# Attention and two MLPs on one core: the first two heads' loads and copies, and the order of the calls at the front and at both changes

## The chip, the cores and the metric

The kernel runs on one core of a Trainium2 chip. The metric is the device time of one launch in microseconds (us), as a median over runs. The launch computes everything, from the inputs in HBM to the output in HBM. The engines are TensorE (PE), VectorE (DVE), ScalarE (ACT), GpSimd (POOL) and SyncE (SP). Each has its own instruction stream, and they meet only in semaphores. SP issues nearly all DMAs, ACT a few.

## The reference

```python
# attention: q, k, v (2, 8, 768, 64), 16 centroids for each of 8 heads
q_assign = argmax(q_n @ c_n)          # nearest centroid of each query, on normed vectors
k_assign = argmax(k_n @ c_n)
mask = q_assign[:, :, :, None] == k_assign[:, :, None, :]
scores = where(mask, scale * q @ k.T, -1e9)
attn = exp(scores - max) / (sum + 1e-9)
x = (attn @ v) as (1536, 512)
# first MLP: w_in (512, 2048), w_out (2048, 512)
h = x @ w_in
x = where(h >= 1, h, where(h <= -1, 0, (h + 1) ** 2 / 4)) @ w_out
# second MLP: w_gate, w_val (512, 1536), w_out (1536, 512)
xn = x / sqrt(mean(x * x) + 1e-6) * rms_g
out = (silu(xn @ w_gate) * (xn @ w_val)) @ w_out
```

All is float32. There are 16 heads in all (2 batches by 8).

## The kernel before

**Numbers.** Matmuls take float32r. A value is split into a high part (a copy rounded to that type) and a low part (the difference), and a product is made from the high and low parts. The splitting is why each PSUM result is read twice: by ACT for the high part, by DVE for the low part.

**Attention, per head of 768 rows in 6 tiles.** Queries and keys of a head lie side by side in `nat` (128 rows by 128 columns a tile). `transpose_qk` transposes the six tiles into PSUM; ACT's `qk_high` writes the high part to `atile`, DVE's `qk_low` the low part to `btile`. In each, rows 0 to 63 are the queries (scaled and negated) and rows 64 to 127 the keys. `assign` multiplies them with the centroids; DVE's `assigned`, `hits` and `masks` and POOL's `rank` turn this into a one-hot mask, which `mask_t` transposes. `assemble` (SP) brings the operands of the scores together: four transfers for the high part (`assemble(True)`), two for the low part (`assemble(False)`), and `send_masks` two for the masks, eight a head, counted in `qk_assembled`. For head 0 ACT issues the low-part transfers (`first_assemble`), and its masks are copied by ACT and DVE without a transfer. `scores` computes one tile of scores, DVE's `cut` takes its extreme values, ACT's `exp` the exponential. `probs_t` transposes the result (nine units a head), `high` (ACT) and `low` (DVE) split it, and `pv` multiplies it with the values.

**Order.** Every engine's order is written out call by call in three places: the front (blocks -3 to 1), the tail of attention with the first steps of the first MLP, and the steps around the change to the second MLP. Between them run loops (`blk`, and `step`). In block n, `probs_t` and `pv` belong to head n, `scores(at(n), t)` to tile t+1 of head n+1 and for t=5 to tile 0 of head n+2, `mask_t`, `assemble` and `send_masks` to head n+2, `transpose_qk` and `assign` to head n+3, and `next_qk` loads head n+4.

**The start.** SP loads head 0's queries, then (`head0.behind()`) the RMS gain, the four pieces of the first up weights and the first down weights, and only then head 1 (which also waits for head 0's loads to land). ACT loads head 0's keys and then the centroids. PE runs `warm(7)`, the transpose of the centroids, `warm(3)`, the transposes of head 0, `warm(4)`, and head 0's assignment; `warm` multiplies ones with ones and its results are not used.

**The MLPs.** The steps run over both MLPs; step s has one pair of column blocks of the up product and one chunk of 512 tokens. An up product is made from seven partial products (`up_part(s, j)`, j = 0 to 6). They are added by DVE's `first_sum`, `second_sum`, `inner_first`, `inner_second`, `second_half` and `first_half` (semaphore `combined`) and ACT's `snap` and `copy_corner`. `bend` and `maximum` (first MLP) or `scale_gate`, `silu` and `product` (second) make the hidden values, `hidden_hi` and `hidden_lo` split them, and `down` multiplies them. PE's order is up(s), down(s-1). The up product's inputs for chunk c are sums of pieces of x, made by POOL (`second_t_sum`, `t_sum`) and split by ACT (`second_t_hi`, `t_hi`) and DVE (`second_t_lo`, `t_lo`). Steps 0 and 1 use chunk 0, steps 2 and 3 chunk 1, whose last parts need the last pair of heads. `up_part(s, 2)` waits for `first_half(s-1)`; `up_part(2, 1)`, `(2, 3)`, `(2, 5)` and `(2, 6)` wait for `second_t_lo` number 7, 8, 9 and 10. Steps 24 on are the second MLP; `take_y` (ACT or DVE) takes a finished down product out of PSUM, and `down` of the next chunk waits for that, one m at a time.

## Time and profile before

| | us |
|---|---|
| median of 3 runs | 818.58 (816.81 to 820.59) |
| the profiled execution | 821.07 |
| its span, first to last instruction | 819.2 |
| PE busy | 801.0 (98%) |
| DVE busy | 639.1 (78%) |
| ACT busy | 490.4 (60%) |
| POOL busy | 402.5 (49%) |

Times of rows are us from the start of the span. Attention fills it to about 270 us, the first MLP from there to about 535, the second the rest. The profiled execution is 1.9 us longer than its span. A busy PE may still be slow: the column PEclk is the clock granted to it, as a share of the full one.

### The profile page before, as it was taken

Reading aid. Unit: us, or ns where it says so; the run is one execution under the profiler, and the core shown is the slowest. Engines: PE = TensorE matmul, PEld = TensorE weight load, DVE = VectorE, ACT = ScalarE, POOL = GpSimd, SP = SyncE. Lnnn points to the kernel's source line nnn. Section 1 sums busy time; section 2 is a strip of 40 time slices with the busy share of each in tenths; the row PEclk is TensorE's granted clock in tenths of the full one; section 3 lists DMA queues with packets and bytes.
Section 4 is the critical chain, followed back from the end, with each engine's and each line's share of the span. In section 5 each row is a group of like instructions: output and inputs, shape, how many; then the busy total and the mean of one; then the engine's idle time right before and its main releaser. Section 6 shows DMA issues by size and latency. Waiting matters only on the chain.

```text
span 819.2 us, 15394 instructions
## 1 busy us (share of the span) xinstructions
PE 801.0 (98%) x5369; PEld 736.0 (90%) x5369; DVE 639.1 (78%) x1221; ACT 490.4 (60%) x894; POOL 402.5 (49%) x356
## 2 busy tenths in 40 slices
PE   7899999999999999999999999999999999999998
PEld 6799999999988889999999899898899999999997
DVE  5799999999997776575665678997767787878666
ACT  2888888888988676655555569877332222222221
POOL 1135443246568853652462465975393673919000
PEclk9999999999999989999999999999999999999999
DMA  8844754755641100200200110200220101110102
GB/s 187 194 108 113 168 131 114 160 125 123 140 109 46 37 1 27 78 1 27 70 8 27 34 45 27 65 26 2 65 66 2 52 1 52 39 27 27 48 31 78
DMA packets 65443, 54.83 MB, mean 67 GB/s; under 512 B 30080, under 2 KB 52608, under 8 KB 65376
## 3 DMA queue, kind: packets, MB, share of 16 engines
q1 hardware_dynamic: 64288, 53.33, 25.5%
q8 instruction: 39, 0.64, 0.3%
q10 hardware_dynamic: 1088, 0.62, 0.3%
q14 instruction: 28, 0.23, 0.1%
HBM read 27.30 MB, written 3.15 MB: 37 GB/s over the span
## 4 chain that ended last, share of the span: by engine, by line
PE 88%; DVE 3%; ACT 3%; DMA 2%; issue 2%; POOL 1%; SPq 1%; ACTq 0%; DVEq 0%; POOLq 0%
PE ps L921 34%; PE ps L949 14%; PE ps L961 12%; PE ps L752 8%; PE ps L735 8%; PE ps L702 4%; PE ps L705 4%; PE ps L770 1%; PE ps L793 1%; PE ps L794 1%; DMA k<-stage 1%; PE ps L816 1%; SPq L536 1%; DVE gl L1930 0%; DMA cnat<-in_centroids 0%
## 5 line engine op out<-in xcount | busy, mean ns | idle before, releaser
L921 PE MATMUL ps<-th,wh 128*128 128x256 f32 x840 | 240.9, 287 | 3.5 <-DVE hid L1904 2.7
L921 PE MATMUL ps<-tl,wh 128*128 128x256 f32 x840 | 239.2, 285 | 0.0
L921 PE MATMUL ps<-th,wl 128*128 128x256 f32 x840 | 239.1, 285 | 0.0
L921 PEld LDWEIGHTS ps<-th,wh 128*128 128x128 f32 x840 | 162.3, 193 | 7.6 <-DVE tl L1732 3.2
L921 PEld LDWEIGHTS ps<-tl,wh 128*128 128x128 f32 x840 | 162.4, 193 | 2.0
L921 PEld LDWEIGHTS ps<-th,wl 128*128 128x128 f32 x840 | 162.3, 193 | 0.0
L2419 POOL TENSOR_TENSOR wl<-wraw,wh 128x448 fp32r<-128x448 f32 x80 | 104.9, 1339 | 1.3
L1745 DVE TENSOR_SCALAR_CACHE_REDUCE sf<-ps 128x768 f32<-128x768 f32 x96 | 91.6, 955 | 15.2 <-PE ps L705 11.8
L1754 DVE TENSOR_TENSOR ptl<-ps,pth 128x512 fp32r<-128x512 f32 x144 | 94.7, 683 | 5.1 <-ACT pth L1163 4.9
L1163 ACT ACTIVATE pth<-ps 128x512 fp32r<-128x512 f32 x144 | 82.8, 588 | 24.8 <-PE ps L752 16.0
L2400 POOL TENSOR_TENSOR wraw<-corner,wraw 128x256 f32<-128x256 f32 x20 | 17.4, 869 | 153.9 <-DMA wraw<-in_moe_w_val 86.0
L1930 DVE TENSOR_TENSOR gl<-hid,gh 128x512 fp32r<-128x512 f32 x84 | 76.0, 910 | 20.1 <-ACT gh L1324 18.6
L1173 ACT ACTIVATE pbuf<-sf,minn 128x768 f32<-128x768 f32 x96 | 89.0, 928 | 1.6 <-DVE sf L1745 0.2
L1300 ACT ACTIVATE hid<-ps 128x256 f32<-128x256 f32 x60 | 22.8, 379 | 106.8 <-PE ps L921 106.8
L735 PE MATMUL ps<-ident,pbuf 128*128 128x128 f32 x576 | 80.6, 274 | 0.5 <-ACT pbuf L1173 0.5
L1913 DVE TENSOR_TENSOR hid<-hid,curve 128x512 f32<-128x512 f32 x48 | 42.6, 888 | 49.0 <-ACT curve L1315 49.0
L949 PE MATMUL ps<-gh,o1h 128*128 128x512 f32 x192 | 75.2, 392 | 0.0
L949 PE MATMUL ps<-gl,o1h 128*128 128x512 f32 x192 | 75.0, 391 | 0.0
L949 PE MATMUL ps<-gh,o1l 128*128 128x512 f32 x192 | 74.8, 390 | 0.0
L735 PEld LDWEIGHTS ps<-ident,pbuf 128*128 128x128 f32 x576 | 68.5, 141 | 6.9 <-DVE ptl L1754 0.7
L1324 ACT ACTIVATE gh<-hid 128x512 fp32r<-128x512 f32 x84 | 52.6, 628 | 36.4 <-DVE hid L1925 27.1
L752 PE MATMUL ps<-pth,vs 128*128 128x512 f32 x192 | 61.9, 363 | 0.0
(149 smaller groups left out, 1778.5 us busy)
## 6 DMA issues: line engine op xcount, KB each, us to landing
q<-atile SPq DMA_DIRECT2D x32, 192.0 KB, 3.4
k<-atile SPq DMA_DIRECT2D x32, 192.0 KB, 3.3
o1raw<-in_moe_w_out SPq DMA_DIRECT2D x8, 512.0 KB, 3.8
nat<-in_q SPq DMA_DIRECT2D x16, 192.0 KB, 4.0
wraw<-in_moe_w_in SPq DMA_DIRECT2D x24, 128.0 KB, 2.6
vnat<-in_v SPq DMA_DIRECT2D x16, 192.0 KB, 3.3
moved<-osb SPq DMA_DIRECT2D x16, 192.0 KB, 4.2
wraw<-in_moe_w_val SPq DMA_DIRECT2D x24, 128.0 KB, 2.6
```

What stands on the lines that cost most here:

```text
L735: last = pe.transpose(w[:, col + t * P:col + (t + 1) * P], pbuf[:, u, first + t, kt * P:(kt + 1) * P], ident[:, :])
L752: last = pe.matmul(ps_o[:, t0 // 4, 0:count * P], vs[:, u, kt, :], part[:, j % 3, col:col + count * P], start=(kt == 0 and i == 0), stop=( ...
L921: last = pe.matmul(dst[:, 0:HC], a[w][:, j, kt, :], b[c][:, j, kt, :], start=(opened and kt == 0 and i == 0), stop=(kt == KH - 1 and i == ...
L949: last = pe.matmul(bank(Y[m]), w[q % 2][:, e, o:o + P], x[b][:, e, :], start=(opens(s) and h == 0 and i == 0), stop=(closes(s) and h == 1 ...
L961: last = pe.matmul(bank(Y[m]), x[b][:, 0, m * P:(m + 1) * P], w[f][:, :], start=(opens(s) and i == 0), stop=(closes(s) and i == 2))
L1163: act.activation(pth[:, j % 3], wbank(PT_AT[j]), ACT.Copy).then_inc(probs_high, 1)
L1173: act.activation(pbuf[:, s, ts, :], sf[:, ts % 2, :], ACT.Exp, bias=minn[:, s, ts:ts + 1], scale=-1.0, accum_out=den[:, s, ts:ts + 1]).the ...
L1324: act.activation(gh[s % 2][:, e, :], half_of(s, e), ACT.Copy).then_inc(hidden_high, 1)
L1745: dve.tensor_scalar(two(sf[:, ts % 2]), score_slot(fixed, t)[:, :, 0:HALF], MASKED, None, ALU.min, ALU.min, accum_out=minn[:, s, ts:ts + 1 ...
L1754: dve.tensor_tensor(ptl[:, j % 3], wbank(PT_AT[j]), pth[:, j % 3].bitcast(F32), ALU.subtract).then_inc(probs_low, 1)
L1930: dve.tensor_tensor(gl[s % 2][:, e, :], half_of(s, e), gh[s % 2][:, e, :].bitcast(F32), ALU.subtract).then_inc(hidden_low, 1)
L2419: pool.tensor_tensor(lo[:, o], raw[:, o], hi[:, o].bitcast(F32), ALU.subtract).then_inc(up_split, 1)
```

## The change

- **Loads.** Head 0's queries and keys are loaded in halves of three tiles: SP loads the first halves (new semaphore `first_half_loaded`), ACT the second halves, behind the centroids. PE's first three transposes wait for the first halves alone. Head 1's load stands next on SP's queue and waits for the second halves.
- **Copies.** For heads 0 and 1 three of the four high-part transfers, those that stay on their partitions, become POOL instructions (`copies`, semaphore `first_copies`); one transfer remains. The scores of heads 0 and 1 and `qk_high` of heads 2 and 3 wait for them, and POOL's first `rank` stands behind all six.
- **Weights.** `head0.behind()` moves from the head of SP's queue to behind head 0's `send_masks`.
- **Orders.** The calls of all engines are reordered in the front; those of ACT, DVE, POOL and SP also at the change from attention to the first MLP (steps 0 to 6) and at the change to the second MLP (steps 19 to 33). `warm` goes from 7, 3, 4, 8 to 6, 0, 5, 2, 8.

The first hunks are SP's and PE's, then ACT's (both changes), DVE's (the first change), and POOL's.

```diff
         def whole(head, parity):
-            return filled(head, parity, DMAS) - (0 if parity else 2 * 16)
+            return filled(head, parity, DMAS) - (3 if parity else 5) * 16
...
-            sp.dma_start(nat[:, 0, :, 0:D], q_v[0]).then_inc(qk_loaded[0], 16)
+            sp.dma_start(nat[:, 0, 0:NT // 2, 0:D], q_v[0][:, 0:NT // 2, :]).then_inc(first_half_loaded, 16)
+            sp.dma_start(nat[:, 0, 0:NT // 2, D:P], k_v[0][:, 0:NT // 2, :]).then_inc(first_half_loaded, 16)
...
                         moves = ((q1[0:D, s], atile[0:D, s]), (k1[0:D, s], atile[D:P, s]),
                                  (k1[D:P, s], atile[D:P, s]), (q2[0:D, s], atile[0:D, s]))
+                        if fixed is not None and fixed < 0:
+                            moves = moves[1:2]
...
-            head0.behind()
             pre3.next_qk()
             pre2.assemble(True)
             pre2.next_qk()
             pre1.assemble(True)
+            pre1.next_v()
+            pre1.assemble(False)
             pre1.next_qk()
             pre2.behind()
-            head0.next_qk()
-            pre1.assemble(False)
             pre1.send_masks()
             head0.assemble(True)
-            pre1.next_v()
+            head0.next_qk()
             head0.assemble(False)
             head0.next_v()
             head0.send_masks()
+            head0.behind()
+            head1.assemble(True)
+            head1.move_half()
+            head1.assemble(False)
+            head1.next_v()
             head1.next_qk()
-            head1.next_v()
-            head1.assemble(True)
-            head1.assemble(False)
-            head1.move_half()
             head1.send_masks()
...
-            warm(7)
+            warm(6)
...
-            warm(3)
...
+                if ts == 0 and number in (0, 1):
+                    pe.wait_ge(first_copies, 3 * (number + 1))
...
-                pe.wait_ge(qk_loaded[s], filled(n + 3, s, 2))
+                if fixed == -3:
+                    pe.wait_ge(first_half_loaded, 2 * 16)
+                else:
+                    pe.wait_ge(qk_loaded[s], filled(n + 3, s, 2))
...
+                    if fixed == -3 and t == NT // 2:
+                        pe.wait_ge(qk_loaded[s], 2 * 16)
...
             transpose_qk(at(-3))
-            warm(4)
+            warm(5)
             assign(at(-3), FIRST)
             assign(at(-3), SECOND)
+            warm(2)
             transpose_qk(at(-2))
...
-            act.dma_start(nat[:, 0, :, D:P], k_v[0]).then_inc(qk_loaded[0], 16)
             act.dma_start(cnat[:, :], cent.rearrange("h c d -> (h c) d")).then_inc(centroids_loaded, 16)
+            act.dma_start(nat[:, 0, NT // 2:NT, 0:D], q_v[0][:, NT // 2:NT, :]).then_inc(qk_loaded[0], 16)
+            act.dma_start(nat[:, 0, NT // 2:NT, D:P], k_v[0][:, NT // 2:NT, :]).then_inc(qk_loaded[0], 16)
...
+                    if fixed in (-1, 0):
+                        act.wait_ge(first_copies, 3 * (fixed + 2))
...
             bend(0, 0)
             snap(1)
-            head16.spread_out()
+            second_t_hi(5, 1)
+            second_t_hi(6, 1)
             hidden_hi(0, 0)
             bend(0, 1)
+            head16.spread_out()
+            hidden_hi(0, 1)
+            bend(1, 0)
+            t_hi(2, 0, 1)
+            t_hi(2, 1, 1)
             copy_corner(1)
-            hidden_hi(0, 1)
-            second_t_hi(5, 1)
-            second_t_hi(6, 1)
             second_t_hi(7, 1)
-            bend(1, 0)
             second_t_hi(8, 1)
...
+            take_y(29, 3)
+            copy_corner(31)
             take_y(29, 2)
-            take_y(29, 1)
-            hidden_hi(30, 0)
-            snap(31)
-            copy_corner(31)
             silu(31)
-            take_y(29, 3)
...
             inner_second(1)
+            second_half(1)
             hidden_lo(0, 1)
             second_t_lo(4, 1)
-            second_half(1)
+            first_half(1)
             second_t_lo(5, 1)
             second_t_lo(6, 1)
             second_t_lo(7, 1)
+            maximum(1, 0)
             second_t_lo(8, 1)
-            maximum(1, 0)
+            first_sum(2)
             second_t_lo(9, 1)
-            first_half(1)
             second_t_lo(10, 1)
-            first_sum(2)
+            second_sum(2)
             hidden_lo(1, 0)
-            second_sum(2)
+            maximum(1, 1)
             inner_first(2)
             inner_second(2)
-            maximum(1, 1)
+            t_lo(2, 0, 1)
+            second_half(2)
             hidden_lo(1, 1)
-            second_half(2)
...
+                def copies():
+                    h, s = n + 2, u
+                    pool.wait_ge(qk_high_done, h + 1)
+                    if fixed == -2:
+                        pool.wait_ge(first_masks_cleared, 1)
+                    else:
+                        pool.wait_ge(first_copies, 3)
+                    for i, (dst, own) in enumerate(((q1, slice(0, D)), (k1, slice(D, P)), (q2, slice(0, D)))):
+                        if i:
+                            pool.wait_ge(first_copies, 3 * h + i)
+                        pool.tensor_scalar(dst[own, s], atile[own, s].bitcast(F32), 1.0, 0.0, ALU.mult, ALU.add)\
+                            .then_inc(first_copies, 1)
...
+                        if fixed == -2:
+                            pool.wait_ge(first_copies, 6)
...
+            pre2.copies()
+            pre1.copies()
             pre2.rank()
```

## Rows read from the trace of the kernel before

**Rows 1.** The page, part 1: busy us (share of the span) xinstructions.
```profile
PE 801.0 (98%) x5369; PEld 736.0 (90%) x5369; DVE 639.1 (78%) x1221; ACT 490.4 (60%) x894; POOL 402.5 (49%) x356
```
**Rows 2.** Windows: us, busy PE, PEld, DVE, ACT, POOL, PEclk, DMA share, GB/s.
```profile
20.00:30.00 10.00, 7.95 (x54) 6.87 (x54) 7.93 (x20) 8.29 (x14) 2.10 (x3) 1.00 1.00 200
30.00:40.00 10.00, 9.09 (x56) 8.64 (x57) 7.56 (x18) 7.20 (x13) 0.00 (x0) 0.83 0.83 207
...
100.00:200.00 100.00, 99.87 (x720) 93.06 (x719) 92.88 (x196) 84.57 (x159) 40.12 (x41) 1.00 0.54 125
...
500.00:550.00 50.00, 49.80 (x329) 45.57 (x328) 46.96 (x76) 39.05 (x71) 38.93 (x29) 1.00 0.17 49
550.00:600.00 50.00, 48.40 (x337) 44.53 (x335) 37.04 (x68) 26.74 (x51) 26.28 (x23) 1.00 0.10 28
```
**Rows 3.** Waits of PE: total us, times, longest us.
```profile
PE ps L921 <- DVE hid L1904: 2.7, 1, 2.7
...
PE ps L702 <- DMA k<-stage: 1.7, 1, 1.7
...
PE ps L961 <- ACT xr L1388: 1.0, 1, 1.0
```
**Rows 4.** The chain of waits over the first 60 us: start, us, what.
```profile
1.49 4.06 DMA cnat<-in_centroids
...
15.95 3.92 DMA nat<-in_k
...
25.50 5.38 DMA k<-stage
```
**Rows 5.** Timeline of the front: start, us, engine, line, output<-input, [idle before <-releaser].
```profile
9.79 1.59 PE L670 MATMUL ps<-ones 128*128 128x512 f32 x4
11.22 0.19 PE L793 MATMUL ps<-cb,atile 128*128 128x64 f32 x1
...
15.17 1.01 DVE L1788 SCALAR_TENSOR_TENSOR btile<-ps,fold,atile 128x768 fp32r<-128x768 f32 x1
...
18.23 0.62 PE L702 MATMUL ps<-k,q 128*128 128x384 f32 x2 [0.42 <-DMA q<-atile]
...
23.42 0.74 SPq L536 DMA_DIRECT2D q<-btile  x1
...
28.81 0.96 DVE L1745 TENSOR_SCALAR_CACHE_REDUCE sf<-ps 128x768 f32<-128x768 f32 x1 [0.41 <-ACT pbuf L1173]
...
30.91 0.82 PE L702 MATMUL ps<-k,q 128*128 128x384 f32 x2 [1.70 <-DMA k<-stage]
...
37.16 0.95 DVE L1745 TENSOR_SCALAR_CACHE_REDUCE sf<-ps 128x768 f32<-128x768 f32 x1
```
**Rows 6.** The source views of L2528 and L2549: duration ns min/median/max.
```profile
L2528 POOL TENSOR_SCALAR vs<-vnat x16: 505/512/523, 25.9 to 247.5; 128x384 fp32r<-128x384 f32 x16
...
L2549 POOL TENSOR_TENSOR tpair<-osb,moved x16: 1828/1847/2192, 55.0 to 276.5; 64x768 f32<-64x768 f32 x16
```
**Rows 7.** Timelines of DVE and ACT at the change to the first MLP.
```profile
282.06 2.39 DVE L1732 TENSOR_TENSOR tl<-traw,th 128x256 fp32r<-128x256 f32 x3
...
287.67 0.41 DVE L1904 TENSOR_TENSOR hid<-ps,snap 128x256 f32<-128x256 f32 x1
...
282.44 0.42 ACT L1152 ACTIVATE th<-traw 128x256 fp32r<-128x256 f32 x1 [1.93 <-POOL traw L2483]
```
**Rows 8.** Windows: the stretch behind the wait of 2.7 us.
```profile
290.00:295.00 5.00, 5.00 (x27) 4.91 (x26) 3.44 (x6) 2.10 (x4) 5.00 (x4) 0.60 0.01 2
```
**Rows 9.** The chain of waits at the change to the first MLP.
```profile
288.23 6.36 PE ps L921 x30
...
300.08 5.03 PE ps L921 x42
```
**Rows 10.** The source view of L1919, and the timeline of POOL.
```profile
L1919 DVE TENSOR_TENSOR hid<-hid,z x36: 683/693/1925, 531.7 to 809.4; 128x512 f32<-128x512 f32 x36
...
589.11 1.70 POOL L2410 TENSOR_SCALAR wh<-wraw 128x1792 fp32r<-128x1792 f32 x1
```

More of the change, by code:

```diff
@@ L623, in _ @@
             load_up(3)
+            load_up(4)
             load_out1(2)
-            load_up(4)
             load_out1(3)
@@ L1517, in _ @@
             t_hi(2, 3, 1)
+            hidden_hi(2, 0)
+            take_y(1, 2)
+            snap(3)
+            take_y(1, 3)
             t_hi(2, 4, 1)
-            take_y(1, 2)
-            hidden_hi(2, 0)
-            snap(3)
             bend(2, 1)
-            take_y(1, 3)
+            copy_corner(3)
+            t_hi(2, 5, 1)
             hidden_hi(2, 1)
-            t_hi(2, 5, 1)
+            bend(3, 0)
             t_hi(2, 6, 1)
-            copy_corner(3)
-            bend(3, 0)
             snap(4)
@@ L1553, in _ @@
             hidden_hi(6, 1)
+            take_y(5, 2)
             for s in range(7, 19):
@@ L1580, in _ @@
             t_hi(3, 1, 1)
-            t_hi(3, 2, 1)
             bend(21, 1)
@@ L1685, in _ @@
             silu(32)
+            hidden_hi(32, 0)
             snap(33)
-            hidden_hi(32, 0)
             copy_corner(33)
+            take_y(32, 0)
+            silu(33)
             take_y(32, 1)
-            silu(33)
             take_y(32, 2)
-            take_y(32, 0)
+            take_y(32, 3)
             hidden_hi(33, 0)
-            take_y(32, 3)
             for s in range(34, NS):
@@ L2041, in _ @@
             head0.low(6)
+            head0.cut(4)
             head0.low(7)
-            head0.cut(4)
-            head1.masks()
             head0.low(8)
             head0.cut(5)
+            head1.masks()
             head1.low(0)
@@ L2171, in _ @@
             maximum(5, 0)
+            maximum(5, 1)
             first_sum(6)
@@ L2174, in _ @@
             second_sum(6)
-            maximum(5, 1)
             inner_first(6)
@@ L2178, in _ @@
             second_half(6)
+            first_half(6)
             hidden_lo(5, 1)
-            first_half(6)
             take_y(5, 0)
+            maximum(6, 0)
             take_y(5, 1)
-            maximum(6, 0)
             maximum(6, 1)
@@ L2221, in _ @@
             take_y(19, 1)
+            take_y(19, 2)
             maximum(20, 1)
-            take_y(19, 2)
+            take_y(19, 3)
             add_squares(0, 0)
-            take_y(19, 3)
             first_sum(21)
             second_sum(21)
+            hidden_lo(20, 0)
             inner_first(21)
-            hidden_lo(20, 0)
+            inner_second(21)
             hidden_lo(20, 1)
-            inner_second(21)
             add_squares(0, 1)
@@ L2235, in _ @@
             first_half(21)
+            add_squares(0, 2)
+            t_lo(3, 1, 1)
             maximum(21, 0)
-            add_squares(0, 2)
-            maximum(21, 1)
             first_sum(22)
             second_sum(22)
+            maximum(21, 1)
+            hidden_lo(21, 0)
             inner_first(22)
-            t_lo(3, 1, 1)
-            hidden_lo(21, 0)
             inner_second(22)
+            hidden_lo(21, 1)
             second_half(22)
-            sums_lo(0)
-            hidden_lo(21, 1)
             t_lo(3, 2, 1)
-            first_half(22)
             t_lo(3, 3, 1)
             t_lo(3, 4, 1)
+            first_half(22)
+            t_lo(3, 5, 1)
+            sums_lo(0)
             maximum(22, 0)
-            t_lo(3, 5, 1)
+            take_y(21, 0)
+            take_y(21, 2)
+            take_y(21, 3)
+            take_y(21, 1)
             maximum(22, 1)
-            hidden_lo(22, 0)
-            take_y(21, 1)
             first_sum(23)
-            take_y(21, 2)
-            take_y(21, 0)
             second_sum(23)
             inner_first(23)
-            take_y(21, 3)
+            hidden_lo(22, 0)
+            inner_second(23)
             hidden_lo(22, 1)
-            inner_second(23)
+            second_half(23)
             inverse(0)
-            second_half(23)
             add_squares(1, 0)
-            add_squares(1, 1)
             first_half(23)
@@ L2271, in _ @@
             maximum(23, 0)
-            add_squares(1, 2)
+            maximum(23, 1)
+            add_squares(1, 1)
             first_sum(24)
@@ L2275, in _ @@
             second_sum(24)
-            maximum(23, 1)
+            hidden_lo(23, 1)
             inner_first(24)
             inner_second(24)
-            hidden_lo(23, 1)
             second_half(24)
+            scale_gate(24)
             first_half(24)
+            add_squares(1, 2)
             sums_lo(1)
-            scale_gate(24)
             t_lo(4, 0, 1)
             take_y(23, 1)
+            take_y(23, 3)
             take_y(23, 0)
@@ L2289, in _ @@
             second_sum(25)
+            hidden_lo(24, 0)
             take_y(23, 2)
             inner_first(25)
-            hidden_lo(24, 0)
             inner_second(25)
             second_half(25)
+            first_half(25)
             scale_gate(25)
-            take_y(23, 3)
+            product(25)
             t_lo(4, 1, 1)
-            first_half(25)
-            product(25)
             first_sum(26)
@@ L2328, in _ @@
             first_sum(28)
-            hidden_lo(27, 0)
             second_sum(28)
             inner_first(28)
+            inverse(2)
+            hidden_lo(27, 0)
             inner_second(28)
             second_half(28)
+            first_half(28)
             scale_gate(28)
@@ L2371, in _ @@
             product(31)
-            hidden_lo(31, 0)
             first_sum(32)
@@ L2376, in _ @@
             inner_second(32)
+            hidden_lo(31, 0)
             second_half(32)
```

322 lines of the change are left out of this document (161 added, 161 removed).

## The prediction

> **What bounds the kernel now.** I read the page first: TensorE (PE) is busy for 801.0 of 819.2 us [rows 1]. Only 18.2 us are idle, so anything worth microseconds must remove idle time of PE or time at its low clock. The windows say where both lie [rows 2]. From 100 to 200 us PE is busy 99.87 of 100, so a gain made ahead of it is carried through undiminished. From 20 to 40 us it is idle 2.05 + 0.91 us, and the granted clock in 30 to 40 is 0.83, which takes another 1.7 us (the granted clock is 1.00 at 2.4 GHz and 0.50 at 1.2); the 0.60 of 290 to 295 us [rows 8] shows the same at the change from attention to the first MLP. Third, PE's waits [rows 3] name the long ones: 2.7 us for DVE's L1904, 1.7 us for the mask transfer k<-stage, 1.0 us for ScalarE's L1388. The chain of waits over the front [rows 4] shows 5.38 us of that mask transfer, and 4.06 us of the centroid load ahead of everything.
>
> **Front: the start.** The centroid load is issued first on ScalarE's queue, in the slot that the K load has now (0.76 us instead of 1.49): its landing comes 0.7 us earlier, at about 4.8 us by the same 4.06 us [rows 4]. Two half loads follow it there and the other two halves go by SP; a whole load is there before the centroids are ready for PE, so I cost the halves at nothing. If a half landed a microsecond late, the first transposes would wait that long. With three warm matmuls gone, the transposes follow the centroid transpose at once. But five warm matmuls then stand ahead of the first assignment, still at the slow pace of the start (four now take 1.59 us [rows 5], five 2.0 from 8.2 on), so it starts at about 10.15 us instead of 11.22 [rows 5]: 1.1 us. The warm(2) added later delays head 1's transposes, whose ScalarE copy is awaited only by the DVE instruction at 15.17 [rows 5], 0.9 us after it is there: nothing.
>
> **Front: copies by GpSimd.** Six transfers of 192 KB of the first two heads become six tensor_scalar on 64 partitions by 768. No such row exists. The nearest is L2528, 128x384 in 0.51 us [rows 6]; twice the elements a partition give 1.0 us each. The bounds are 0.5 us (as if partitions counted) and 1.85 us (L2549, 64x768 with two inputs [rows 6]), 1.5 to 5.5 us for three. I take 3 us. Head 0's high part is whole at 8.9 us (the transposes end at 8.2, two ScalarE copies behind), so its copies run to 12. Its first scores come at 16.7: now 18.23 [rows 5], less the 1.1, less 0.4 of a wait for one of the removed transfers. Head 1's run from 13.7 to 16.7, its scores come after 27. Both are hidden, head 0's with 4.7 us to spare. Behind them on GpSimd waits only head 1's ranking, ready at about 17.4. ScalarE's copies for heads 2 and 3 also wait on them, and come at 18.5 and 26.
>
> Against this speaks a row: L1919 of DVE, two SBUF inputs, takes 0.69 us and once 1.93, beside a GpSimd tensor_scalar of 1.70 us [rows 10]. DVE's mask chain has four instructions with two SBUF inputs a head, 0.26 to 0.36 us each. If each start falls on a copy, each waits up to a copy; head 1's copies meet perhaps one or two of head 0's. I count 0.3 us, bounds 0 and 3. The Trainium skill ("SBUF — State Buffer", Who interferes with whom) says the shared port is an exclusive lock between GpSimd and a DVE instruction with two SBUF inputs, held for the whole instruction. L1919 agrees; by that rule alone the term would be a copy for every overlap.
>
> **Front: the queue.** Now SP issues head 1's low-part moves at 23.42 us, though their data is ready at 16.18 (15.17 + 1.01) [rows 5], because loads of heads 2, 3, 4 and v stand ahead. After the change they leave at about 15, head 2's load at about 10 instead of 15.22, and head 4's load behind the masks. Fewer issues and 1 MB of weights less ahead of 30 us shorten every landing. Head 2's K load, landing at 19.87 (15.95 + 3.92 [rows 4]), no longer holds the transposes of 20.00: they start at 17.6, 2.4 us earlier. From there ScalarE's table load and five exponentials run in the old order with hardly a gap, so the last cut of head 0, 28.81 + 0.96 = 29.77 us [rows 5], comes at about 27.35. The masks of head 1 are then long landed (sent at 22.5, landing by 27 even with the old 3.9), so the first scores of head 1 go at 27.45 instead of 30.91 [rows 5]: 3.5 us. The clock drop that now follows the wait of 30 us should go too, 1.7 us. But DVE then sets the pace: by its order the cut of head 1's second tile ends at 34.4 instead of 38.1 (37.16 + 0.95 [rows 5]), 3.7 us. PE has by then done one half assignment more. I take 4.3 less the 0.3 for the port: **4.0 us**. Bounds: 1.1 (only the start) and 5.2 (3.5 + 1.7).
>
> **Weights later.** Six issues of about 0.6 us leave SP behind head 2's masks, at about 31 to 35 us, so they end long before head 1's next move has its data (when PE has ended head 1's scores, after 40). GpSimd sums the first weights only behind head 1's work. Nothing; if the cover were gone, head 3's assembly would be late by 3.5 us at most.
>
> **First change, attention to MLP.** PE's order is the same. Now its up(2) stops before j=2 from 285.5 to 288.23 [rows 3, 9] because j=2 waits for first_half(1), which DVE runs at 287.67, behind six second_t_lo and maximum(1, 0) [rows 7]; its products were done before down(0) began. Then PE runs 30 matmuls in 6.36 us, where 42 take 5.03 us later [rows 9], so 2.8 us go to the clock. In the new order first_half(1) stands behind second_t_lo(4), at about 282. What is late next is j=1: second_t_lo(7) needs the attention output, and ScalarE does bend(1, 0), two t_hi and a corner ahead of its part, so its copy at 282.44 [rows 7] comes at 283.7; j=1 starts at 284.95 instead of 284.5. j=3 waits for second_t_lo(8) behind maximum(1, 0), to 286.95; j=5 and j=6 for the next two, to 289.05. up(2) ends at 289.8 instead of 294.59. down(1) then loses about 1.1 us at its second half (hidden_lo(1, 1) at 293.6). Left: 4.8 - 1.1, **3.6 us** rounded down. It holds only if pieces of idle of 0.5 to 1.1 us do not lower the clock as 2.74 us did. Bounds: 0.8 (clock falls as before) and 5.5 (stall and clock all gone). The spreading of reciprocals is moved behind bend(0, 1), to 279.0; GpSimd's multiplication needs it at 278.88: 0.1 us, inside.
>
> **Second change, MLP to MLP.** PE is idle 0.2 us in 500 to 550 and 1.6 in 550 to 600 (49.80 of 50, 48.40 of 50 [rows 2]). The largest is the 1.0 us wait for ScalarE's L1388 [rows 3]: take_y(29, 3) stands behind silu(31), which waits for the stretched L1919. In the new order take_y(29, 2) and (29, 3) stand ahead of silu(31): 1.0 us off. The rest of the reordering I cannot price but by these rows: **1.0 us**, bounds 1.8 off and 1.5 more, since DVE is busy 46.96 of 50 us there [rows 2]. Attention's loop and the last stages are untouched.
>
> **Sum.** 4.0 + 3.6 + 1.0 = 8.6 us off the profiled run: 821.07 to 812.5 (span 819.2 to 810.6, 1.9 us around it). The profiled run lies 2.5 us above the median of the three timed ones, 818.58, so the forecast is 818.58 - 8.6 = **810.0 us**. Its own range is 806 to 814.
>
> **Rivals.**
> First, the clock still falls at the first change, or j=1 waits longer behind ScalarE's new order: 0.8 there, total 5.8, 812.8 us. For it: three new waits in a row. Against: of PE's waits [rows 3] the 1.7 and the 2.7 are followed by a low clock, the 1.0 is not (the clock of 550 to 600 is 1.00 [rows 2]). Chance 0.16.
> Second, the copies hold DVE by the port, and the front keeps 1.2: total 5.8, also 812.8 us. For it the 1.93 us; against it, the mask chain's instructions are short and mostly beside no copy. Chance 0.08. The rule of the Trainium skill named above would give this too, if nearly every one of them met a copy.
> Third, the transfers were hidden anyway: DVE and ScalarE pace the front, the start gains 1.1, nothing else in the front stays, and the first change gives 0.8: 816.7 us. For it: DVE is busy 7.93 and 7.56 of 10 us from 20 to 40 [rows 2]; against it, the remaining 4.5 us are idle. Chance 0.11.
> Fourth, slower: at the second change DVE's new order delays a sum that PE awaits. DVE has 3 us of slack in 50 there, so one late entry pushes the next. A stall of 2.7 us or more brings the low clock and costs 2.7 + 2.8 = 5.5 us; two of them, 11.0, outweigh the 8.6 and give 821.0. It decides from the second such stall. Against it: PE's waits there are at most 1.0 us now. Chance 0.07.
>
> **Numbers.** The forecast has 0.58. All cases but the last two are below 814.5, which is 0.5% off (about what a measurement of this kernel can tell from no change): faster 0.82, same 0.11, slower 0.07. The range reaches from 805.5 (upper bounds of two terms) to 816.5, leaving out the third rival's far end and the fourth.
>
> **What would show it.** The start: assignment near 10.1 us. The copies: about 1.0 us each, no DVE instruction over 1 us beside them. The queue: no wait of PE for k<-stage, the first scores of head 1 near 27.5, clock 1.00 from 30 to 40. First change: first_half(1) at 282, clock 1.00 at 290 to 295, up(2) ending 4.8 us earlier relative to the end of pv. Second: no wait for L1388. Wrong would make it a low clock anywhere behind 10 us, a PE wait over 2 us, or scores of head 1 after 29.

## Result, and the profile after

The changed kernel took 809.75 us (median of four runs, 807.90 to 812.15) against 819.29 us before (816.81 to 820.59): a ratio of 0.9889, interval 0.9851 to 0.9927. Four more runs of it later gave 810.99 us (808.98 to 812.79), ratio 0.9906 [0.9888, 0.9923]. The forecast was 810.0. The profiled run is 810.72 us with a span of 808.9, so 10.3 us of span have gone. Part 1 of its page, beside [rows 1]:

```profile
PE 796.5 (98%) x5368; PEld 731.7 (90%) x5368; DVE 642.9 (79%) x1221; ACT 489.6 (61%) x894; POOL 406.4 (50%) x362
```

PE's busy time falls by 4.5 us for the same work: matmuls at half clock have become rarer. The windows after, columns as in [rows 2] and [rows 8]:

```profile
20.00:30.00 10.00, 8.10 (x60) 7.19 (x58) 9.19 (x21) 9.52 (x19) 2.12 (x3) 1.00 0.35 83
30.00:40.00 10.00, 10.00 (x72) 9.42 (x71) 9.65 (x21) 7.53 (x16) 1.15 (x3) 1.00 1.01 231
285.00:290.00 5.00, 3.65 (x16) 2.67 (x16) 4.38 (x7) 3.80 (x7) 4.92 (x4) 1.00 0.01 2
290.00:295.00 5.00, 5.00 (x40) 4.79 (x39) 2.52 (x6) 4.15 (x9) 5.00 (x4) 1.00 0.02 3
550.00:600.00 50.00, 50.00 (x353) 46.92 (x352) 35.07 (x65) 23.89 (x47) 26.99 (x25) 1.00 0.15 38
690.00:700.00 10.00, 9.51 (x61) 8.41 (x60) 9.86 (x14) 1.92 (x4) 9.67 (x10) 1.00 0.01 2
```

From 30 to 40 us PE is busy throughout and at full clock (before: 9.09 at 0.83); at 290 it is at full clock (before 0.60); the DMA share of 20 to 30 is down from 1.00 to 0.35. The last row is new: idle time in a stretch that nobody edited. PE's waits, beside [rows 3]:

```profile
PE ps L708 <- DVE sf L1760: 1.5, 2, 0.8
PE ps L960 <- DVE gl L1945: 1.4, 1, 1.4
...
PE ps L932 <- DVE pair L1897: 0.5, 1, 0.5
```

The 2.7 us, the 1.7 us for k<-stage and the 1.0 us for the xr line are gone. The front, beside [rows 5] (timeline; L804 was L793, L1794 makes head 0's masks, L2594 is the new copy, L708 was L702, L1760 was L1745):

```profile
3.77 0.24 ACT L1144 ACTIVATE ccat<-cnat 128x64 f32<-128x64 f32 x1
5.55 1.49 PE L781 MATMUL ps<-ident,nat 128*128 128x128 f32 x6
8.97 0.26 PE L804 MATMUL ps<-cb,atile 128*128 128x64 f32 x1
12.95 1.06 DVE L1794 TENSOR_TENSOR masks<-ramp,m 128x96 fp32r<-128x96 f32 x2
12.99 0.91 POOL L2594 TENSOR_SCALAR q<-atile 64x768 fp32r<-64x768 f32 x1 [2.50 <-ACT atile L1215]
16.41 0.59 PE L708 MATMUL ps<-k,q 128*128 128x384 f32 x2
27.18 0.58 PE L708 MATMUL ps<-k,q 128*128 128x384 f32 x2 [0.71 <-DVE sf L1760]
32.70 0.96 DVE L1760 TENSOR_SCALAR_CACHE_REDUCE sf<-ps 128x768 f32<-128x768 f32 x1 [0.16 <-ACT pbuf L1186]
```

The first change, timelines of DVE and PE (L1919 is first_half, L1973 t_lo, L1945 hidden_lo):

```profile
276.70 0.41 DVE L1919 TENSOR_TENSOR hid<-ps,snap 128x256 f32<-128x256 f32 x1
...
285.28 1.11 DVE L1973 TENSOR_TENSOR tl<-xr,th 128x512 fp32r<-128x512 f32 x1
286.32 0.41 DVE L1915 TENSOR_TENSOR hid<-ps,snap 128x256 f32<-128x256 f32 x1
286.65 1.43 DVE L1945 TENSOR_TENSOR gl<-hid,gh 128x512 fp32r<-128x512 f32 x1
...
288.14 0.50 PE L960 MATMUL ps<-gh,o1h 128*128 128x512 f32 x1 [1.35 <-DVE gl L1945]
```

first_half(1) is done at 277.11, 3.2 us before PE reaches the products that read it (280.29), so nothing waits for it; the new wait is for hidden_lo(1, 1), behind t_lo(2, 0) and second_half(2).

Relative to the product that follows attention, up(2) ended 5.5 us earlier than before, and the new wait took 1.6 us of that back with what follows it.

To say where time went, I matched the 2520 weight products of the MLPs (L921, now L932) by number in each trace and compared their starts with before's. Gain in us of each stretch: "front" is up to product 1 (259.06 us before), "change 1" to product 128 (up(3) runs), "middle" to 981 (513.46), "change 2" to 1471 (617.64), "late" to 2101 (734.34).

```
kernel           front  change 1  middle  change 2   late   sum
after             5.02     3.86    -0.23     2.86   -1.21  10.30
after_again       6.41     3.91     0.28     2.38   -0.96  12.02
front_only        6.48    -0.16     0.08     0.04   -1.22   5.22
change1_only     -2.38     4.03    -1.21    -0.21    0.00   0.23
change2_only      0.89    -0.62    -0.17     2.85    0.00   2.95
first_half_only  -0.04     3.43     0.24     1.78   -1.20   4.21
late_first_half   5.81     2.23     0.12     2.40   -1.36   9.20
no_copies         1.95     4.04     0.24    -0.05    0.00   6.18
old_queue         6.44     3.88     0.44     2.40   -1.18  11.98
weights_early    -0.55     3.96     0.15     2.85    0.00   6.41
whole_loads       5.92     4.04    -0.44     2.40    0.00  11.92
centroids_last    4.87     3.88    -0.23     0.50    0.00   9.02
both_better       6.13     5.52    -0.67     2.38   -0.01  13.35
```

### The profile page after: what moved, and what is told of

Its sections match the earlier page's. It is cut to its first block, busy times and chain, and to the rows that moved or that the text cites. A ratio compares the mean times of both kernels' runs of the same rounds, so it can differ in the third digit from the quotient of the medians.

```text
span 808.9 us, 15399 instructions
## 1 busy us (share of the span) xinstructions
PE 796.5 (98%) x5368; PEld 731.7 (90%) x5368; DVE 642.9 (79%) x1221; ACT 489.6 (61%) x894; POOL 406.4 (50%) x362
## 4 chain that ended last, share of the span: by engine, by line
PE 93%; DVE 3%; ACT 2%; issue 1%; ACTq 0%; DVEq 0%
PE ps L932 36%; PE ps L960 16%; PE ps L972 12%; PE ps L758 8%; PE ps L741 8%; PE ps L708 5%; PE ps L711 4%; PE ps L804 1%; PE ps L805 1%; PE ps L781 1%; PE ps L827 1%; PE ps L725 1%; ACT pbuf L1186 1%; DVE gl L1945 0%; DVE hid L1928 0%
## 5 line engine op out<-in xcount | busy, mean ns | idle before, releaser
L932 PE MATMUL ps<-th,wh 128*128 128x256 f32 x840 | 239.1, 285 | 0.7 <-DVE pair L1897 0.5
L932 PE MATMUL ps<-th,wl 128*128 128x256 f32 x840 | 237.7, 283 | 0.0
L932 PE MATMUL ps<-tl,wh 128*128 128x256 f32 x840 | 237.7, 283 | 0.0
L932 PEld LDWEIGHTS ps<-th,wh 128*128 128x128 f32 x840 | 160.9, 192 | 4.4 <-DVE pair L1897 1.0
L932 PEld LDWEIGHTS ps<-tl,wh 128*128 128x128 f32 x840 | 161.0, 192 | 2.0
L932 PEld LDWEIGHTS ps<-th,wl 128*128 128x128 f32 x840 | 160.9, 192 | 0.0
L1760 DVE TENSOR_SCALAR_CACHE_REDUCE sf<-ps 128x768 f32<-128x768 f32 x96 | 91.6, 954 | 12.8 <-PE ps L711 9.5
L1945 DVE TENSOR_TENSOR gl<-hid,gh 128x512 fp32r<-128x512 f32 x84 | 74.8, 895 | 16.6 <-ACT gh L1339 15.2
```

Of the source, the lines that this page charges most:

```text
L932: last = pe.matmul(dst[:, 0:HC], a[w][:, j, kt, :], b[c][:, j, kt, :], start=(opened and kt == 0 and i == 0), stop=(kt == KH - 1 and i == ...
L1760: dve.tensor_scalar(two(sf[:, ts % 2]), score_slot(fixed, t)[:, :, 0:HALF], MASKED, None, ALU.min, ALU.min, accum_out=minn[:, s, ts:ts + 1 ...
L1945: dve.tensor_tensor(gl[s % 2][:, e, :], half_of(s, e), gh[s % 2][:, e, :].bitcast(F32), ALU.subtract).then_inc(hidden_low, 1)
```

## Experiments

**One part at a time.** Three kernels take one of the three parts each, the fourth a single call.

front_only: the kernel before with the front alone (half loads, copies, SP's front order, weights later, warm matmuls). Of its edit:

```diff
-            head0.behind()
             pre3.next_qk()
...
+            head0.behind()
...
+            pre2.copies()
+            pre1.copies()
```

> The kernel before with the front alone changed (loads, copies, weights, warm, orders up to head 1); both changes in the old order. If the parts add up: attention ends 5.0 us earlier (the last pv at 264.4 instead of 269.5), the stall of 2.7 us and the low clock at the first change stay, and the time falls by 5.0 us. Rival, the untouched steps give part of it back because DVE and GpSimd meet at other moments: the same 5.0 at the end of attention, but less than 3.5 at the end.

Measured 815.84 us against 818.65 before, ratio 0.9973 [0.9952, 0.9995]. Its trace has PE busy all of 30 to 40 us at clock 1.00 and keeps the first change's wait, with a clock of 0.66 from 280 to 290. The median fell by 2.8 us, not by 5.0, as the rival had it; of the 6.48 us that the trace gains at the end of attention, 1.22 are given back behind 690 us.

change1_only: the edits at the change from attention to the first MLP alone. Of DVE's:

```diff
             second_t_lo(4, 1)
-            second_half(1)
+            first_half(1)
...
-            first_half(1)
```

> The kernel before with the calls at the change from attention to the first MLP alone reordered. If the gain there comes from the order alone: up(3) starts 3.9 us earlier than in the kernel before (296.2 instead of 300.1), granted clock 1.00 from 290 to 295 us, time 3.9 us less. Rival, it needs the earlier front: a stall of over 2 us stays, the clock falls, and the gain is at most 1 us.

Measured 817.23 us, ratio 0.9972 [0.9954, 0.9989]. Its traced change 1 is 4.03 us faster at clock 1.00, the long wait gone, so the order alone does it there. The median fell by 1.4 us only.

change2_only: the edits from the end of the first MLP on alone. Of ScalarE's:

```diff
-            scale_x(0, 0, 1)
-            snap(21)
             squares(0, 2, 1)
-            scale_x(0, 1, 1)
+            snap(21)
+            scale_x(0, 0, 1)
...
+            scale_x(0, 1, 1)
```

> The kernel before with the calls at the change to the second MLP alone reordered. If the order alone does it: no wait of PE for take_y, and 2.4 us less between up(29) and up(35). Rival, a part of these 2.4 is the chance of where GpSimd's long instructions meet DVE's scale_gate: only the 1.0 us of the wait is gone, and the rest moves by up to 1 us either way.

Measured 818.07 us, ratio 0.999 [0.9971, 1.001], which does not tell it from no change. The trace gains 2.85 us at change 2, with no wait for take_y, and keeps the first change's wait, now 3.3 us, with a clock of 0.62 from 290 to 295.

first_half_only:

```diff
             second_half(1)
+            first_half(1)
             second_t_lo(5, 1)
...
-            first_half(1)
```

> The kernel before with one call moved: DVE's first_half(1) from behind second_t_lo(9) to ahead of second_t_lo(5). If the clock is the larger part and one long stall causes it: the wait of 2.7 us splits into pieces under 1.4 us, the granted clock stays 1.00, and the gain is about 4 us, as much as the whole reordering there. Rival, the clock falls all the same, since PE idles for about as long in sum: gain at most 1 us.

Measured 815.85 us, ratio 0.998 [0.9958, 1.0002], an interval that still holds 1. The timeline of PE and the windows:

```profile
288.30 0.36 PE L921 MATMUL ps<-th,wh 128*128 128x256 f32 x1 [1.24 <-ACT snap L1294]
```
```profile
290.00:295.00 5.00, 4.80 (x25) 4.07 (x25) 3.17 (x7) 3.10 (x6) 5.00 (x4) 1.00 0.00 2
```

One call gives 3.43 of the 3.9 us in the trace, leaving a wait of 1.2 us for ScalarE.

The three parts' medians add up to 4.8 us, less than the 8.2 to 9.5 of the whole, while their traces in their own stretches (6.48, 4.03, 2.85) add up to more than the whole. In their own stretches the three parts do not hinder each other. Why the medians add up to less is not shown. Two things work that way: the traced gains are taken against one execution of before, 821.07 us, which lies 2.4 us above this median of before, and the unedited stretches behind a part can give time back, as shown below.

**What each front edit carries.** All four are the changed kernel with one thing put back.

no_copies:

```diff
-                        if fixed is not None and fixed < 0:
-                            moves = moves[1:2]
...
-            pre2.copies()
-            pre1.copies()
```

> The changed kernel (809.75 us, first product of the output stage at 254.04 us in its profile) with GpSimd's six copies taken out and the six transfers of 192 KB put back, everything else of the change kept (half loads, order of SP, weights later). Theory, copies matter: the three transfers of head 1 stand in SP's queue again, each of 0.5 to 1.0 us of issue, ahead of the low-part moves and the masks, and 1 MB more is moved ahead of 30 us; head 1's first scores come 1.5 to 3 us later than 27.18, PE waits over 1 us for k<-stage, with a lower clock behind it: stage end 2 to 4 us later, 811.7 to 813.7 us. Rival, the order of the queue alone has done it: head 1's first scores stay within 0.7 us of 27.18, clock 1.00 from 30 to 40 us, and the mask chain loses its wait beside the copy (two mask instructions in about 0.45 us instead of 1.06), so the time is 809.0 to 810.3 us.

Measured 812.73 us, ratio 0.993 [0.9907, 0.9953], 1.7 and 3.0 us over the two medians of the changed kernel, with intervals that overlap. But the theory named the wrong place: PE has no wait for a transfer. Its timeline shows what took 3 us of front in this trace:

```profile
12.39 1.48 PE L777 MATMUL ps<-ident,nat 128*128 128x128 f32 x6
13.52 3.76 PE L673 MATMUL ps<-ones 128*128 128x512 f32 x8
```

These are the matmuls of 0.82 and 2.08 us in the changed kernel: PE stayed at the slow pace to 17 us. None of these lies behind a wait that the changed kernel does not have. change1_only, with the front of before, shows the same 3.76 us, so this comes with and without the edit. Nor is the change 2 loss of 2.9 us one of the copies: it is a wait of 1.55 us at 532 us in code that the edit does not touch, the same that centroids_last has (below). What the copies are worth stays open, between 0 and about 3 us. That GpSimd's copies are hidden is shown: PE never waits for them.

old_queue:

```diff
-            pre1.next_v()
-            pre1.assemble(False)
             pre1.next_qk()
             pre2.behind()
+            head0.next_qk()
+            pre1.assemble(False)
             pre1.send_masks()
             head0.assemble(True)
-            head0.next_qk()
+            pre1.next_v()
```

> The changed kernel with the order of SP's queue of before for head 1: its low-part moves and its masks go behind the loads of head 4 and v, as they did; copies by GpSimd, half loads and later weights are kept. Theory, the queue is what held head 1: its low-part moves leave some 3 us later than 15.0 us and the masks behind head 4's loads, the first scores of head 1 come at 28.5 to 30 instead of 27.18, PE waits 1 to 2.5 us ahead of them: 811 to 813.5 us. Rival, with three transfers fewer the queue is short enough in any order: the scores within 0.5 us of 27.18 and the time within 1 us of 809.75.

Measured 811.36 us, ratio 0.9924 [0.9898, 0.9949]; front 6.44 against 6.41 in after_again, head 1's first scores at 25.74 in both. The rival held: with three transfers fewer a head and no weights, this reordering carries nothing. The issue of head 1's low parts comes at 18.03, not 23.42 [rows 5], in the old order too.

weights_early:

```diff
+            head0.behind()
             pre3.next_qk()
...
-            head0.behind()
```

> The changed kernel with the six weight loads (the last part of SP's steps for head 0) back ahead of head 0's moves, where they were before the change. Theory of the prediction: no wait of PE hangs on them, within 0.5 us of 809.75. Rival: 3.6 us of issue and 0.75 MB stand ahead of the moves of heads 2 and 3 and of the masks of head 1, the masks land after 27 us, and the first scores of head 1 wait 1 to 3 us, with a low clock behind: 811 to 813.5 us.

Measured 812.79 us, ratio 0.993 [0.9905, 0.9956]. Of the three front edits put back here, it is the one that makes a new DMA wait. PE's timeline and two windows:

```profile
5.45 0.82 PE L781 MATMUL ps<-ident,nat 128*128 128x128 f32 x6
12.19 1.51 PE L781 MATMUL ps<-ident,nat 128*128 128x128 f32 x6 [2.30 <-DMA nat<-in_k]
13.35 3.76 PE L675 MATMUL ps<-ones 128*128 128x512 f32 x8
```
```profile
10.00:20.00 10.00, 7.81 (x40) 6.96 (x41) 4.00 (x9) 1.70 (x2) 2.81 (x4) 0.66 0.89 181
20.00:30.00 10.00, 9.40 (x51) 8.28 (x49) 8.21 (x19) 6.85 (x12) 2.13 (x3) 0.74 0.23 52
```

Head 1's K load, issued at 5.68 behind six weight loads, landed at about 12.1 us; PE idled 2.3 us and then ran at half clock. The wait is at head 1's transposes, not at the masks, as the rival had it. Its size in the median, 1.8 and 3.0 us over the changed kernel's two, is the rival's, but the intervals overlap. The trace shows 7.0 us of front against after_again, and the edit is not shown to be the cause of all of it: the clock fell a second time, to 0.51 from 24.8 to 28.2 us, behind a wait of 0.4 us that after_again has too.

late_first_half:

```diff
             second_t_lo(4, 1)
-            first_half(1)
...
+            second_t_lo(9, 1)
+            first_half(1)
             first_sum(2)
-            second_t_lo(9, 1)
```

> The changed kernel with one call of DVE back where it was: first_half(1) behind the tenth part of the MLP input's low half instead of the fifth. Theory, this call's place makes the stall and the low clock: PE waits 2 to 2.7 us at its first half again, clock 0.5 to 0.8 in some 5 us behind it, the start of up(3) 3.4 to 4.0 us later (first_half_only gained 3.41 us at that place), 813 to 814 us if the other parts keep theirs. Rival, the rest of the reordering (maximum(1, 0), first_sum(2), ScalarE's new order) carries half of it: 1.5 to 2 us later, clock 1.00.

`second_t_lo(9, 1)` thus comes ahead of `first_sum(2)` as well. Measured 812.73 us, ratio 0.9928 [0.9905, 0.9951]: 1.7 us over after_again, with overlapping intervals; in the trace, change 1 gains 2.23 instead of 3.9. PE's waits:

```profile
PE ps L960 <- DVE gl L1945: 2.0, 1, 2.0
...
PE ps L932 <- DVE hid L1919: 0.7, 1, 0.7
```

The rival held. With the rest of the reordering in place the call's late place costs 1.7 us, and the clock stays at 1.00 there: the stall is split into 0.72 and 2.01 us, with 6.6 us between them.

**The start, a control, and a better version.**

after_again: no edit.

> The changed kernel once more, without any edit, as the base of the three kernels run with it. Expected 808.5 to 811 us by its four earlier runs (807.90 to 812.15). Its profile tells whether the 1.2 us that the changed kernel gave back between 692 and 708 us (DVE's scale_gate at 1.78 and 2.04 us beside GpSimd) is met again: theory, it hangs on where GpSimd's long instructions fall, so it returns wherever the kernel runs 5 us or more ahead of before at that place; rival, a chance event of one execution, gone in this one.

Measured 810.99 us. The loss behind 690 us came back, 0.96 us. The theory that a lead of 5 us decides is false all the same: whole_loads, centroids_last and both_better are 9.0 to 13.4 us ahead there and lose nothing; front_only, 6.44 ahead, loses 1.22, and weights_early, 6.41 ahead, nothing. Two lines of this control's timeline show another thing:

```profile
5.45 0.82 PE L781 MATMUL ps<-ident,nat 128*128 128x128 f32 x6
...
7.84 0.27 PE L804 MATMUL ps<-cb,atile 128*128 128x64 f32 x1 [0.41 <-DVE btile L1809]
```

The same kernel ran the same transposes in 0.82 us here and 1.49 us in the first trace.

whole_loads:

```diff
-            sp.dma_start(nat[:, 0, 0:NT // 2, 0:D], q_v[0][:, 0:NT // 2, :]).then_inc(first_half_loaded, 16)
...
+            sp.dma_start(nat[:, 0, :, 0:D], q_v[0]).then_inc(qk_loaded[0], 16)
...
-            act.dma_start(nat[:, 0, NT // 2:NT, 0:D], q_v[0][:, NT // 2:NT, :]).then_inc(qk_loaded[0], 16)
...
+            act.dma_start(nat[:, 0, :, D:P], k_v[0]).then_inc(qk_loaded[0], 16)
```

> The changed kernel with head 0's first loads whole again: q of 192 KB by SyncE, k of 192 KB by ScalarE behind the centroids, in place of four halves. The start gained 2.25 us (first assignment 8.97 instead of 11.22 us) where 1.1 us were forecast. Theory A, the order of ScalarE's queue did it (centroids first): the centroids still come at 3.8 us, K whole is issued at 1.2 and lands near 5.2 us, the first assignment stays at 8.9 to 9.4 us, the time within 0.7 us of the changed kernel. Theory B, the smaller transfers did it, by shortening the centroids' landing (2.3 us instead of 4.1): centroids again at about 4.8 us, first assignment at about 10 us, 1 us more in all. Theory C, the halves matter by their own landing: K whole lands after 6 us, the first transposes wait 0.5 us or more for it, 0.5 to 1.5 us more.

Measured 810.64 us, ratio 0.991 [0.9877, 0.9943]: theory A, with the first assignment at 8.44 us, even earlier than it said. ScalarE, with one issue fewer, starts its table load at 1.88 instead of 2.37 us and its first work on the centroids at 3.29 instead of 3.77; the transposes start at 5.08, with no wait for K. The halves bring nothing.

centroids_last:

```diff
-            act.dma_start(cnat[:, :], cent.rearrange("h c d -> (h c) d")).then_inc(centroids_loaded, 16)
             act.dma_start(nat[:, 0, NT // 2:NT, 0:D], q_v[0][:, NT // 2:NT, :]).then_inc(qk_loaded[0], 16)
             act.dma_start(nat[:, 0, NT // 2:NT, D:P], k_v[0][:, NT // 2:NT, :]).then_inc(qk_loaded[0], 16)
+            act.dma_start(cnat[:, :], cent.rearrange("h c d -> (h c) d")).then_inc(centroids_loaded, 16)
```

> The changed kernel with ScalarE's three first issues in the other order: both half loads, then the centroids. They are issued at 1.85 instead of 0.75 us. Theory, the start hangs on the centroids alone, and their landing is at least 2.3 us behind the issue: they come at 4.3 to 4.9 us, first assignment 9.5 to 10.2 instead of 8.97, 0.5 to 1.2 us more in all. Rival, the table load (to 3.66 us) and the half loads pace the start in either order: within 0.3 us.

Measured 811.72 us, ratio 0.9907 [0.9884, 0.9929]. ScalarE's timeline:

```profile
4.63 0.26 ACT L1144 ACTIVATE ccat<-cnat 128x64 f32<-128x64 f32 x1 [0.77 <-DMA cnat<-in_centroids]
```

The first assignment came at 9.53 instead of 8.97 us, 0.56 us later, as the theory has it. Only 0.15 us of this is lost at the end of the front, but the two traces do not compare cleanly: PE reached its full pace at 9.1 us here and at 9.8 in the first trace, so the assignment ended only 0.18 us later (10.79 against 10.61). What the order costs beyond the start is not settled.

both_better:

```diff
-            t_lo(2, 0, 1)
-            second_half(2)
             hidden_lo(1, 1)
+            second_half(2)
+            t_lo(2, 0, 1)
...
                         pool.wait_ge(first_copies, 3)
+                        pool.wait_ge(mask_made, 2)
```

> The changed kernel with two calls moved: DVE's hidden_lo(1, 1) ahead of t_lo(2, 0) and second_half(2), against the 1.35 us that PE waits at down(1)'s second half; and GpSimd's copies of head 1 behind head 0's masks, against the 0.63 us that the mask instructions lose beside the first copy. Theory: the wait at down(1) falls to 0.3 us (1 us gained), the masks take 0.45 instead of 1.06 us and the front gains 0.3 to 0.6 us: 1.3 us less in all, about 808.4 if the changed kernel has 809.7. Rival, both are taken back: second_half(2) comes 1.1 us later and up(3) waits for it, and the copies of head 1 then meet head 0's other DVE work: within 0.5 us of the changed kernel.

`second_half(2)` now also runs ahead of `t_lo(2, 0)`. Measured 810.98 us, ratio 0.9906 [0.9875, 0.9937]. In its trace both steps do what they should. DVE's timeline:

```profile
12.41 0.43 DVE L1794 TENSOR_TENSOR masks<-ramp,m 128x96 fp32r<-128x96 f32 x2
...
284.17 1.00 DVE L1945 TENSOR_TENSOR gl<-hid,gh 128x512 fp32r<-128x512 f32 x1
```

The masks take 0.43 us instead of 1.06, PE has no wait at down(1), change 1 gains 5.52 instead of 3.9, and its span of 805.9 us is the shortest. But its five runs lie between 807.65 and 814.55, with the control's median. A version that beats the changed kernel was not shown.

## Why the prediction was right, and where its steps were not

**Start, 1.1 us: too small.** It was 2.25 us (8.97 instead of 11.22 [rows 5]). The forecast kept the 4.06 us of landing [rows 4]; issued first, the centroids landed in 2.3 us, in 2.8 when issued third (centroids_last), in 1.8 with whole loads. ScalarE then waited for its own table load instead. The loads in halves, costed at nothing, bring nothing (whole_loads). "Still at the slow pace" was true of the first trace (five warm matmuls in 2.48 us) and false of five others of this start (1.41 us): there the start gained 3.4 us. So the size of this term hangs on the execution.

**Copies.** Hidden, as forecast: 0.83 us each instead of 1.0, head 0's over at 10.5 and head 1's at 15.7 us. The port term was 0.3 us; it was 0.63 on DVE, since the masks at 12.95 met the copy at 12.99, with a wait of 0.25 on PE behind it. "No DVE instruction over 1 us beside them" held narrowly: one mask instruction took 0.88 us instead of 0.26. both_better, with the copy behind the masks, shows 0.43 for both, so this meeting is the cause. This agrees with the Trainium skill ("SBUF — State Buffer", Who interferes with whom): DVE with two SBUF inputs and GpSimd exclude each other on the shared port. In both_better head 0's scores follow 5.31 us behind the end of its assignment (10.07 to 15.38) and not 5.80 (10.61 to 16.41), so the meeting cost about 0.5 us.

**Queue.** The result was forecast well: head 1's first scores at 27.18 (27.45), the masks sent at 22.1, no wait for k<-stage, clock 1.00 from 30 to 40, the second cut at 33.66 (34.4). In part this was luck: 2.25 us of the 3.7 at head 1's first scores are the start's, so the rest gained 1.5 us (1.8 in after_again) where 2.4 were forecast. The reason given, the new order of SP's queue, carries nothing (old_queue). Which of the other edits took the wait for k<-stage away is not shown: it is absent in no_copies and weights_early too, and even in change2_only, where PE waits 1.4 us for head 2's K load instead. The number of warm matmuls and the new orders of PE, ScalarE and DVE in the front were not tried alone.

**Weights later, 0: looked at one side only.** That nothing waits for the weights in their new place held. What the step left out is what they hold up in their old one. In the kernel before, head 1's K load behind them landed at 10.1 us and its transposes began at 12.48, so the late start covered it; with the new start it is awaited 2.3 us (weights_early, one trace, in which it landed at 12.1). The forecast credited fewer bytes to the queue's term, for head 2's load, and named no wait at head 1's, so the total does not show the omission.

**The front altogether** gained 5.0 us in the first trace and 5.0 to 6.5 over the four traces of the unedited front, against 4.0 forecast; three of the four are over the bound of 5.2.

**First change, 3.6 us: right.** 3.9 us, with the wait of about 1.1 us at down(1) found as 1.35. first_half(1) was called the cause; alone it brings 3.43, but put back it costs only 1.7, so the rest of the new order would have brought 2.2 without it. The condition on the clock held at this change: it fell behind waits of 2.74 and 3.3 us (0.60, 0.62) and not behind 1.35 or 2.01. The length of a wait does not decide it everywhere, though. The windows of 20 to 30 us of late_first_half and of after_again, two kernels that are the same up to there:

```profile
20.00:30.00 10.00, 9.29 (x56) 8.43 (x55) 8.73 (x20) 9.23 (x17) 1.81 (x3) 0.83 0.40 95
```
```profile
20.00:30.00 10.00, 8.51 (x61) 7.64 (x62) 9.28 (x20) 9.29 (x18) 1.82 (x3) 1.00 0.47 104
```

Up to 21 us both have the same waits within 0.02 us, the last of 0.41 us at 19.2. In late_first_half the clock then fell to half for some 3 us, in after_again it stayed. It also fell at 27.0 us in change1_only behind 0.41 us, and at 20.8 in change2_only behind 1.37. Why is open.

**Second change, 1.0 us: the priced part held, the rest is partly not its own.** PE's wait for take_y is in three of the four traces without these edits (1.0 to 1.3 us) and in none of the ten with them, though scale_gate is stretched there as well (1.72 us at 588.6 in change2_only). So the new order takes it away, as forecast. In eight of the ten the whole stretch gains 2.4 to 2.9 us, in two 0.5 and 0, and the median of change2_only shows no gain. And first_half_only, which has none of the edits, gains 1.78 there, 1.2 of it at that wait. Why the wait is missing, its timeline shows beside [rows 10], DVE's scale_gate and GpSimd:

```profile
585.80 0.69 DVE L1919 TENSOR_TENSOR hid<-hid,z 128x512 f32<-128x512 f32 x1
```
```profile
585.82 2.24 POOL L2410 TENSOR_SCALAR wh<-wraw 128x1792 fp32r<-128x1792 f32 x1
```

Before, GpSimd began its 1.70 us at 589.11, scale_gate 0.31 us behind it took 1.93, and PE waited 1.0 us. Here DVE began 0.02 us ahead: scale_gate took 0.69, GpSimd 2.24, and PE waited for nothing there. In these two meetings the one that was first paid nothing. In centroids_last a meeting with GpSimd ahead, stretching `hidden_lo` to 1.85 us (0.89 in the first trace, where DVE was ahead), stands in the chain of waits that leads to 1.55 us of idle PE, in a kernel whose MLP code is the changed kernel's. GpSimd's, DVE's and PE's timeline:

```profile
517.01 2.03 POOL L2425 TENSOR_SCALAR wh<-wraw 128x1792 fp32r<-128x1792 f32 x1
517.73 1.85 DVE L1945 TENSOR_TENSOR gl<-hid,gh 128x512 fp32r<-128x512 f32 x1
...
530.02 0.38 PE L932 MATMUL ps<-th,wh 128*128 128x256 f32 x1 [1.55 <-DVE pair L1897]
```

**What was not forecast: 1.2 us given back.** In the first trace, DVE's and PE's timeline behind 688 us:

```profile
688.98 1.78 DVE L1934 TENSOR_TENSOR hid<-hid,z 128x512 f32<-128x512 f32 x1
691.67 1.49 DVE L1940 TENSOR_TENSOR hid<-hid 128x512 f32<-128x512 f32 x1
693.86 1.70 DVE L1945 TENSOR_TENSOR gl<-hid,gh 128x512 fp32r<-128x512 f32 x1
...
695.95 0.38 PE L932 MATMUL ps<-th,wh 128*128 128x256 f32 x1 [0.48 <-DVE pair L1897]
```

Three DVE instructions of 0.7 us when alone take 5 us together beside GpSimd (busy 9.67 of 10), and PE runs dry. A loss of 0.95 us or more in this stretch occurred in six of fourteen traces, at leads of 5 to 13 us, and not in the rest. In [rows 10] and first_half_only, a shift of 0.3 us between the two engines changed the outcome. No run settled what sets the draw.

**The sum.** 4.0 + 3.6 + 1.0 = 8.6 stands against 5.02 + 3.86 - 0.23 + 2.86 - 1.21 = 10.3 of the first trace. The medians moved 8.2 and 9.5, since the profiled run of before, at 821.07, lies some 2 us above its median, as the prediction said. Errors of both signs met: the start and the second change were too small, what the queue brings was too large, and the loss behind 690 us was missing. That the median came out at 809.75 against 810.0 is therefore luck in part. Of the range, the lower end of 805.5 does not come out of the stated bounds: all three upper ones give 12.5 us off, 806.1.

## What to carry to other kernels

When a start is pulled forward, recheck every transfer that was covered by its lateness: the loads ahead of the next one in the queue can become the wait. At the first change a long wait of PE cost its own length plus the low clock behind it, and splitting or shortening it saved both; short waits are no guarantee of a full clock, as late_first_half shows. Where DVE and GpSimd are both near full, small moves anywhere earlier redraw their meetings for 1 to 3 us, so judge an edit by its own stretch in the trace, and by medians of many runs.

## What the runs showed of the hardware

- PE's pace at the start differs between executions with the same instructions: six transposes at 5.5 us took 0.82 or 1.49 us. The slow pace (eight 128x512 matmuls in 3.76 us instead of 2.08) is that of the lower clock level, 1.2 GHz. The windows read 1.00 there all the same, because a trace holds no record of the clock before its first rise to full. That first record stands at 4.0 to 4.6 us in six traces, at 8.4 to 10.7 in six (9.8 in the first trace, 10.7 in before), and at 17.4 (no_copies) and 20.1 (change1_only) in two, and PE's durations change at these times. It is worth up to 3 us of front.
- A GpSimd tensor_scalar fp32 to fp32r of 64x768 takes 0.83 us, and 0.91 when it meets DVE.
- Runs of one kernel, all at a granted clock of 0.999 or 1.00, spread over 7 us (both_better). One trace each cannot say why.
